# Attention and two dense networks on one core: three buffers of probabilities, and the first chunk in another order

## The chip, the cores and the metric

The kernel runs on one core of a Trainium2 chip. The metric is the device time of one execution in microseconds. Three runs of the kernel before gave 484.89, 485.83 and 486.81 us; the median, 485.83, is the number to be compared with.

## The reference

Three stages, all in float32. First a local attention with a summary of everything: 2 batches, 8 heads, 768 positions, 64 elements per head. Each query sees the keys less than 16 positions away and, beside them, 24 summary keys, one for every block of 32 (the maximum of the block's keys; the summary's value is the mean of the block's values).

```python
k_sum = k.reshape(B, H, nb, block, D).max(axis=3)
v_sum = v.reshape(B, H, nb, block, D).mean(axis=3)
scores_s = scale * np.einsum('bhsd,bhnd->bhsn', q, k_sum) + np.log(block)
scores_all = np.concatenate([np.where(mask_l, scale * (q @ k.T), -1e9), scores_s], axis=-1)
a = np.exp(scores_all - max); a = a / (sum(a) + 1e-9)
attn = a @ np.concatenate([v, v_sum], axis=2)
...
x = np.maximum(x @ w_in, 0.0) ** 2 @ w_out            # 1536 x 512 -> 2048 -> 512
...
h = x @ w_in2; solu = h * softmax(h)                  # 512 -> 1024
out = ((solu - mean) / sqrt(var + 1e-6) * g_ln) @ w_out2
```

## The kernel before, in words

**The attention.** The work is cut into 32 units (`UNITS`); a unit is a pair of heads and three tiles of 64 queries, and four units (`PPB`) with the same rows cover the four pairs of a batch. Eight units (`UPC`) give 384 tokens, a chunk; there are four chunks. A unit u goes through these steps, each a small function on the engine that does it:

- `windows_k` (GpSimd, L372) and `summaries_k` (GpSimd, L384) lay the keys of the three windows and the 24 summaries into `k_ext`; the summaries come from `sums_k` (VectorE, L593).
- `scores` (TensorE, L810): twelve small matmuls in the first chunk, three in the later ones.
- `maxima` (VectorE, L611): scale and mask into `probs[:, u % 2]` (L621), then the row maxima (L625).
- `exps` (ScalarE, L438): three exponentials in place (L443).
- `reciprocals` and `normalise` (VectorE, L628 and L635).
- `turned` (TensorE, L840): three transpositions into PSUM (L850); `copy_probsT` (ScalarE, L447) copies them to SBUF.
- `values` (TensorE, L863): twelve matmuls of the probabilities with `v_ext_first` (first chunk) or `v_ext` (L880).
- `x_high` (ScalarE, L454) and `x_low` (VectorE, L642) write the result as two parts, a high one rounded to the fast matmul format and the remainder.

The means of the first batch's values are matmuls too: `means` (L853) multiplies `v_first` by a column matrix, `copy_mean` (L465) copies the result into `v_ext_first`. Those of the second batch are made by `sums_v` and `mean_v` (L601, L606) in the steady loop and spread by DMA (`spread_v`, L267).

**The first network.** Each float32 product is three fast matmuls (high x high, high x low, low x high). For each of 16 hidden tiles f, `up` (L910, in quarters `up_part`, L897) multiplies 4 x 3 times into one PSUM bank, `hidden` makes relu and square on ScalarE (L488) and VectorE (L648), `down` (L923) multiplies 4 x 3 times by w_out. The high parts of a weight tile are made by `w_in_high` and `w_out_high` on ScalarE (L472, L476), the low parts by `w_in_low` and `w_out_low` on VectorE (L659, L664), except the first two tiles of w_in, whose low parts GpSimd makes (L392).

**The order.** Every engine has a list written out by hand for the first eight units and the first steps of the network: SyncE's requests L286 to L318, GpSimd L397 to L419, ScalarE L503 to L541, VectorE L688 to L736, TensorE L944 to L985. Waiting instructions hold up everything behind them on the same engine. TensorE's list ends with `turned(8)` and `scores(9)`; then comes the steady loop (L986), whose first product is `up(2)` and in which the later units' attention is put into slots between `up` and `down`. Some idle matmuls (`keep_busy`, L939) stand ahead of the first scores.

All loads go through one queue, in the order of the requests: keys, first queries, mask, identity, `v_first` for four pairs, `v_ext_first` in two halves (`load_vw_first`, one for each set of rows, 576 KB), and then later queries, windows of values and the weights in groups of two tiles (`load_w`).

The waits that matter here: `maxima(u)` waits for `probsT_ps` of unit u-2, since it writes into that unit's buffer; `scores(u)` waits for `masked_ok` of unit u-2 (two PSUM banks); `turned(u)` for the copy of unit u-2; `values(u)` for the mean of its pair, for `copy_probsT(u)`, for `x_low(u-2)` and, at the first unit of four, for the windows of values (`vwf_in`).

Of the kernel before, what the change touches and what calls it, by code (L numbers as in the profile page):

```python
# [7 lines left out]
F32 = mybir.dt.float32  # L8
# [71 lines left out]
def build(nc, qT, q_head, kT, vrows, vblk, vwin, vwin_head, w_in_t, w_out_t, w2_t, g_cols, mask_c, ident_c, y_dram, out):  # L80
    ctx = ExitStack()
    with ctx:
# [47 lines left out]
        v_mean = sb(att, "v_mean", [PPB * NB, P], F32)  # L130
# [3 lines left out]
        probs = sb(att, "probs", [P, 2, UC], F32)  # L134
        probsT = sb(att, "probsT", [P, 2, TPU * P], F32)
        neg_max = sb(att, "neg_max", [P, 2, TPU], F32)
        row_sum = sb(att, "row_sum", [P, 2, TPU], F32)
        row_den = sb(att, "row_den", [P, 2, TPU], F32)
        row_rec = sb(att, "row_rec", [P, 2, TPU], F32)
# [22 lines left out]
        qf_in, vwf_in = [sem(f"qf_in{i}") for i in range(3)], [sem(f"vwf_in{h}") for h in range(HPC)]  # L162
# [18 lines left out]
        win_hi_ok, win_lo_ok, win_low_ok = sem("win_hi_ok"), sem("win_lo_ok"), sem("win_low_ok")  # L181
# [67 lines left out]
        def _(sp):  # L249
# [17 lines left out]
            def spread_v(p):  # L267
                src = v_mean[p * NB:(p + 1) * NB, :].unsqueeze(1).to_broadcast([NB, TPU, P])
                sp.dma_start(v_ext[0:NB, p, :].rearrange("p (t d) -> p t d", t=TPU), src).then_inc(vs_in[p], 16)
# [13 lines left out]
            def load_vw_first(h):  # L283
                sp.dma_start(v_ext_first[NB:KX, h, :], vwin_head[h, :, :]).then_inc(vwf_in[h], 16)
# [22 lines left out]
            for u in range(UPC + 1, UPC + PPB):  # L307
                load_q(u)
                load_vw(u)
# [61 lines left out]
        def _(pool):  # L371
# [20 lines left out]
            def w_in_low(f):  # L392
                pool.wait_ge(win_hi_ok, f + 1)
                nc.gpsimd.tensor_tensor(win_lo[:, tile_cols(f)], win_raw[:, tile_cols(f)],
                                        win_hi[:, tile_cols(f)].bitcast(F32), ALU.subtract).then_inc(win_lo_ok, 1)

# [16 lines left out]
            w_in_low(1)  # L413
# [23 lines left out]
        def _(act):  # L437
            def exps(u):  # L438
                act.wait_ge(max_ok, u + 1)
                s = u % 2  # L440
# [62 lines left out]
            exps(0)  # L503
            copy_probsT(0)
            exps(1)
            exps(2)
            copy_mean(0)
            copy_mean(1)
            w_in_high(0)
            copy_probsT(1)  # L510
            w_in_high(1)
            exps(3)
            exps(4)
            copy_probsT(2)
            copy_mean(2)
            x_high(0)
            copy_probsT(3)
            x_high(1)
            exps(5)
            copy_mean(3)  # L520
            copy_probsT(4)
            x_high(2)
            exps(6)
            x_high(3)
            copy_probsT(5)
            x_high(4)
            exps(7)
            copy_probsT(6)
            x_high(5)
            w_out_high(0)  # L530
            x_high(6)
            copy_probsT(7)
            w_in_high(2)
            x_high(7)
            exps(8)
            hidden(0)
            hidden(1)
            copy_probsT(8)
            w_in_high(3)
            exps(9)  # L540
            w_out_high(1)  # L541
# [50 lines left out]
        def _(dve):  # L592
# [14 lines left out]
            def mean_v():  # L607
                dve.wait_ge(vsum_ok, VP)
                nc.vector.tensor_scalar_mul(v_mean[:, :], v_sum[:, :], 1.0 / BLOCK).then_inc(vavg_ok, 1)

            def maxima(u):  # L611
                row = u // PPB % RB
                s, kind = u % 2, 0 if row == 0 else 2 if row == RB - 1 else 1
# [5 lines left out]
                if u >= 2:  # L619
                    dve.wait_ge(probsT_ps, u - 1)  # L620
# [7 lines left out]
            def reciprocals(u):  # L628
                s = u % 2
# [5 lines left out]
            def normalise(u):  # L635
                s = u % 2
# [56 lines left out]
            reciprocals(0)  # L693
            normalise(0)
            maxima(1)
# [4 lines left out]
            reciprocals(2)  # L700
            normalise(2)
            maxima(3)
            maxima(4)
            reciprocals(3)
            normalise(3)
            reciprocals(4)
            normalise(4)
            maxima(5)
            x_low(0)
            maxima(6)  # L710
            x_low(1)
            reciprocals(5)
            normalise(5)
            x_low(2)
# [4 lines left out]
            x_low(4)  # L719
            reciprocals(7)  # L720
            normalise(7)
            x_low(5)
            x_low(6)
            maxima(8)
            x_low(7)
            w_in_low(2)
            reciprocals(8)
            normalise(8)
            hidden(0)
            w_out_low(0)  # L730
            maxima(9)
            hidden(1)
            reciprocals(9)
            normalise(9)
            w_in_low(3)
            w_out_low(1)  # L736
            for n in range(STEPS):
# [68 lines left out]
        def _(pe):  # L806
# [33 lines left out]
            def turned(u):  # L840
# [8 lines left out]
                for t in range(TPU):  # L849
                    last = nc.tensor.transpose(turned_bank(u, t), probs[:, u % 2, t * KX:(t + 1) * KX], ident[:, 0:P])  # L850
# [280 lines left out]
```

## Time and profile before

| what | before |
|---|---|
| median of three runs | 485.83 us |
| the profiled execution | 485.56 us |
| its span, first to last instruction | 483.8 us |
| TensorE busy | 474.5 us, 98% |
| VectorE busy | 254.0 us, 52% |
| ScalarE busy | 207.6 us, 43% |
| GpSimd busy | 32.8 us, 7% |

The times of rows and stretches count from the start of the span. A row of the timeline has its start, its length, engine, line, operation, output and inputs, and in brackets how long the engine was idle ahead of it and what ended that. Matmuls overlap, so the length of a group is a little more than the step from it to the next.

### The profile page before, as it was taken

The page shows a single profiled execution, that of the slowest core. Times are in us where ns is not written, and L with a number is a line of the kernel's source. Part 1 is how long each engine was busy: PE and PEld are TensorE (multiplying, and loading weights), DVE is VectorE, ACT ScalarE, POOL GpSimd, SP SyncE. Part 2 cuts the span into 40 slices and gives each one's busy share as a digit, 9 for nine tenths or more (in the row PEclk, how much of TensorE's full clock was granted, in tenths as well). Part 3 has the DMA queues.
Part 4 walks back from the last instruction along what each step waited for, and adds up shares of the span by engine and source line. Part 5 has one row for each costly group of instructions (what it writes and reads, how often), then busy time and mean ns, then how long its engine had stood idle before and what let it go on. Part 6 is the DMA issues. An engine that isn't in the chain of part 4 may idle for free.

```text
span 483.8 us, 7841 instructions
## 1 busy us (share of the span) xinstructions
PE 474.5 (98%) x2990; PEld 436.1 (90%) x2990; DVE 254.0 (52%) x515; ACT 207.6 (43%) x525; POOL 32.8 (7%) x62
## 2 busy tenths in 40 slices
PE   7899999999999999999999999999999999999997
PEld 5689999999999999999999999999888888888885
DVE  5779787985444444544443334456674444444450
ACT  3887575553534334433343323334353333333341
POOL 3420000330000000000000000000000000000000
PEclk9999999999999999999999999999999999999999
DMA  8999433222300110401000412121122000000001
GB/s 307 301 335 355 130 96 90 68 91 79 123 29 30 41 47 30 158 31 54 5 1 1 132 43 88 43 88 44 48 84 66 22 24 29 32 28 22 23 22 45
DMA packets 27270, 39.73 MB, mean 82 GB/s; under 512 B 2560, under 2 KB 16800, under 8 KB 27232
## 3 DMA queue, kind: packets, MB, share of 16 engines
q1 hardware_dynamic: 27232, 39.22, 25.0%
q8 instruction: 24, 0.39, 0.3%
q14 instruction: 14, 0.11, 0.1%
HBM read 32.77 MB, written 6.29 MB: 81 GB/s over the span
## 4 chain that ended last, share of the span: by engine, by line
PE 86%; issue 7%; DMA 2%; DVE 2%; SPq 1%; ACT 1%; POOL 0%; POOLq 0%; ACTq 0%; DVEq 0%
PE bank L933 25%; PE bank L903 25%; PE bank L1055 12%; PE bank L1028 12%; PE bank L825 4%; PE bank L880 3%; DMA v_first<-vrows 2%; PE bank L850 2%; PE bank L1043 2%; PE bank L859 1%; DVE solu L783 1%; DVE stat L775 1%; DVE lnT_lo L796 0%; SPq L251 0%; PE bank L831 0%
## 5 line engine op out<-in xcount | busy, mean ns | idle before, releaser
L903 PE MATMUL bank<-x_hi,win_hi 128*128 128x384 f32 x256 | 87.8, 343 | 0.0
L933 PE MATMUL bank<-h_hi,wout_hi 128*128 128x384 f32 x256 | 85.9, 336 | 0.0
L903 PE MATMUL bank<-x_hi,win_lo 128*128 128x384 f32 x256 | 85.8, 335 | 0.0
L933 PE MATMUL bank<-h_hi,wout_lo 128*128 128x384 f32 x256 | 85.7, 335 | 0.0
L903 PE MATMUL bank<-x_lo,win_hi 128*128 128x384 f32 x256 | 85.7, 335 | 0.0
L933 PE MATMUL bank<-h_lo,wout_hi 128*128 128x384 f32 x256 | 85.6, 334 | 0.0
L652 DVE TENSOR_TENSOR sqr<-relu 128x384 f32<-128x384 f32 x64 | 35.7, 558 | 88.1 <-ACT relu L492 87.8
L492 ACT ACTIVATE relu<-bank 128x384 f32<-128x384 f32 x64 | 31.5, 492 | 109.0 <-PE bank L903 109.0
L903 PEld LDWEIGHTS bank<-x_hi,win_hi 128*128 128x128 f32 x256 | 48.2, 188 | 0.4 <-DVE win_lo L661 0.2
L903 PEld LDWEIGHTS bank<-x_lo,win_hi 128*128 128x128 f32 x256 | 48.2, 188 | 0.0
L933 PEld LDWEIGHTS bank<-h_lo,wout_hi 128*128 128x128 f32 x256 | 48.1, 188 | 0.0
L933 PEld LDWEIGHTS bank<-h_hi,wout_hi 128*128 128x128 f32 x256 | 48.1, 188 | 0.0
L933 PEld LDWEIGHTS bank<-h_hi,wout_lo 128*128 128x128 f32 x256 | 48.1, 188 | 0.0
L903 PEld LDWEIGHTS bank<-x_hi,win_lo 128*128 128x128 f32 x256 | 48.1, 188 | 0.0
L775 DVE TENSOR_REDUCE stat<-bank 128x1 f32<-128x1024 f32 x12 | 14.7, 1225 | 49.1 <-PE bank L1028 49.1
L570 ACT ACTIVATE e_sb<-bank,stat 128x1024 f32<-128x1024 f32 x12 | 13.4, 1117 | 61.3 <-DVE stat L775 61.3
L443 ACT ACTIVATE probs<-probs,neg_max 128x120 f32<-128x120 f32 x96 | 36.5, 382 | 7.2 <-DVE neg_max L625 7.1
L1055 PE MATMUL bank<-win_hi,lnT_hi 128*128 128x512 f32 x96 | 38.4, 400 | 0.0
L656 DVE TENSOR_TENSOR h_lo<-sqr,h_hi 128x384 fp32r<-128x384 f32 x64 | 36.1, 564 | 4.2
L1055 PE MATMUL bank<-win_hi,lnT_lo 128*128 128x512 f32 x96 | 37.5, 391 | 0.0
L1055 PE MATMUL bank<-win_lo,lnT_hi 128*128 128x512 f32 x96 | 37.4, 390 | 0.0
L452 ACT COPY probsT<-bank 120x384 f32<-120x384 f32 x32 | 15.2, 476 | 45.6 <-PE bank L850 45.4
(79 smaller groups left out, 725.1 us busy)
## 6 DMA issues: line engine op xcount, KB each, us to landing
q_sb<-qT SPq DMA_DIRECT2D x24, 192.0 KB, 2.8
win_raw<-w_in_t SPq DMA_DIRECT2D x8, 512.0 KB, 11.7
wout_raw<-w_out_t SPq DMA_DIRECT2D x8, 512.0 KB, 12.4
win_raw<-w_t SPq DMA_DIRECT2D x8, 512.0 KB, 3.2
v_ext<-vwin SPq DMA_DIRECT2D x24, 144.0 KB, 2.8
k_raw<-kT SPq DMA_DIRECT2D x8, 400.0 KB, 4.0
out<-o_sb SPq DMA_DIRECT2D x12, 256.0 KB, 2.0
v_first<-vrows SPq DMA_DIRECT2D x4, 384.0 KB, 9.2
```

Source lines behind the costliest of these rows:

```text
L443: last = nc.scalar.activation(probs[:, s, c], probs[:, s, c], ACT.Exp, bias=neg_max[:, s, t:t + 1], accum_out=row_sum[:, s, t:t + 1])
L452: nc.scalar.copy(probsT[0:KX, u % 2, :], src).then_inc(probsT_ok, 1)
L492: nc.scalar.activation(relu[:, n % 2, :], up_bank(n), ACT.Relu).then_inc(relu_ok, 1)
L652: nc.vector.tensor_tensor(sqr[:, n % 3, :], relu[:, n % 2, :], relu[:, n % 2, :], ALU.mult)\
L656: nc.vector.tensor_tensor(h_lo[:, n % 3, :], sqr[:, n % 3, :], h_hi[:, n % 3, :].bitcast(F32), ALU.subtract).then_inc(hlo_ok, 1)
L775: nc.vector.tensor_reduce(stat[:, p, 0:1], h2_bank(s), AX.X, ALU.max, negate=True).then_inc(m2_ok, 1)
L825: last = nc.tensor.matmul(out_[:, t * KX:(t + 1) * KX], q_sb[:, p, t * P:(t + 1) * P], k_ext[:, p, t * KX:(t + 1) * KX], start=True, stop= ...
L880: last = nc.tensor.matmul(out_[e * D:(e + 1) * D, t * QT:(t + 1) * QT], v_tile(u, t, e), probsT[0:KX, u % 2, t * P + e * QT:t * P + (e + 1 ...
L903: last = nc.tensor.matmul(up_bank(n), win[a][:, f * WC + k * P:f * WC + (k + 1) * P], x[b][:, c % 2, k * CH:(k + 1) * CH], start=(k == 0 a ...
L933: last = nc.tensor.matmul(down_bank(d), wout[a][:, f * WC + d * P:f * WC + (d + 1) * P], h[b][:, n % 3, :], start=(f == 0 and a == 0 and b ...
L1028: last = nc.tensor.matmul(bank[:, (0, 6)[p] + half, :], y_tile(s, a, k), w2[b][:, (k * FH + half) * WC:(k * FH + half + 1) * WC], start=(k ...
L1055: last = nc.tensor.matmul(bank[:, 4 + p, :], ln[a][:, p, f * P:(f + 1) * P], w2[b][:, (F2 + f) * WC:(F2 + f + 1) * WC], start=(f == 0 and ...
```

## The change

The buffer `probs` and the four small ones beside it (`neg_max`, `row_sum`, `row_den`, `row_rec`) get three parts in place of two, and every index `u % 2` into them becomes `u % 3`; `maxima(u)` waits for the transposition of unit u-3. `v_mean` goes; `mean_v` writes `v_sum` in place and `spread_v` reads that. GpSimd's `w_in_low` goes, and VectorE makes the low parts of all tiles of w_in. `v_ext_first` is loaded in four requests (two for each set of rows, two pairs each) and `values(u)` waits for its own at each even unit. The lists of all five engines for the first chunk are put in another order, and `up_part` waits for `x_low` in front of `up(1)` too.

```diff
-        v_mean = sb(att, "v_mean", [PPB * NB, P], F32)
-        probs = sb(att, "probs", [P, 2, UC], F32)
+        probs = sb(att, "probs", [P, 3, UC], F32)
...
-        qf_in, vwf_in = [sem(f"qf_in{i}") for i in range(3)], [sem(f"vwf_in{h}") for h in range(HPC)]
+        qf_in, vwf_in = [sem(f"qf_in{i}") for i in range(3)], [sem(f"vwf_in{g}") for g in range(UPC // 2)]
...
-            def load_vw_first(h):
-                sp.dma_start(v_ext_first[NB:KX, h, :], vwin_head[h, :, :]).then_inc(vwf_in[h], 16)
+            def load_vw_first(g):
+                h, cols = g // 2, slice((g % 2) * 2 * TPU * P, (g % 2 + 1) * 2 * TPU * P)
+                sp.dma_start(v_ext_first[NB:KX, h, cols], vwin_head[h, :, cols]).then_inc(vwf_in[g], 16)
...
             load_vf(1)
+            sp.dma_start(q_first[:, 1, :], q_head[1, :, :]).then_inc(qf_in[2], 16)
             load_w(win_raw, w_in_t, 0, win_in)
-            sp.dma_start(q_first[:, 1, :], q_head[1, :, :]).then_inc(qf_in[2], 16)
             load_vw_first(0)
+            load_vw(UPC)
             load_vf(2)
-            load_vw_first(1)
             load_vf(3)
             load_q(UPC)
+            load_vw_first(1)
+            load_vw_first(2)
             sp.dma_start(mask[:, UC + KX:], mask_c[:, UC + KX:]).then_inc(edge_in, 16)
+            load_q(UPC + 1)
+            load_vw(UPC + 1)
+            load_vw_first(3)
+            load_q(UPC + 3)
+            load_w(win_raw, w_in_t, 1, win_in)
             load_w(wout_raw, w_out_t, 0, wout_in)
-            load_w(win_raw, w_in_t, 1, win_in)
-            load_vw(UPC)
-            for u in range(UPC + 1, UPC + PPB):
-                load_q(u)
-                load_vw(u)
+            load_q(UPC + 2)
+            load_vw(UPC + 3)
+            load_vw(UPC + 2)
             load_w(wout_raw, w_out_t, 1, wout_in)
...
             windows_k(0)
             summaries_k(0, 0)
+            windows_k(1)
             summaries_k(0, 1)
-            windows_k(1)
             windows_k(2)
             summaries_k(0, 2)
             windows_k(3)
+            summaries_k(0, 3)
             windows_k(4)
             windows_k(5)
-            summaries_k(0, 3)
             windows_k(6)
             windows_k(7)
-            w_in_low(0)
-            w_in_low(1)
...
-                if u >= 2:
-                    dve.wait_ge(probsT_ps, u - 1)
+                if u >= 3:
+                    dve.wait_ge(probsT_ps, u - 2)
...
-                    if p == 0:
-                        pe.wait_ge(vwf_in[row], 16)
+                    if u % 2 == 0:
+                        pe.wait_ge(vwf_in[u // 2], 16)
...
-                if f == 0:
+                if f == 0 or n == 1:
                     pe.wait_ge(xlo_ok, c * UPC + (HPC - 1) * PPB + k + 1)
```

The new lists of the three engines that compute, up to the loop (r, n, m for `reciprocals`, `normalise`, `maxima`; c for `copy_probsT`):

```
ScalarE: exps(0) exps(1) copy_mean(0) exps(2) c(0) copy_mean(1) w_in_high(0) exps(3)
 c(1) exps(4) x_high(0) exps(5) x_high(1) c(2) copy_mean(2) w_in_high(1) c(3)
 copy_mean(3) x_high(2) c(4) exps(6) x_high(3) x_high(4) c(5) exps(7) x_high(5) c(6)
 w_in_high(2) x_high(6) c(7) exps(8) x_high(7) w_out_high(0) hidden(0) w_in_high(3)
 c(8) w_out_high(1) hidden(1) exps(9)
VectorE (behind sums_k(0,2) r(0)): m(1) n(0) m(2) sums_k(0,3) r(1) n(1) r(2) m(3) n(2)
 m(4) m(5) r(3) x_low(0) n(3) r(4) n(4) r(5) n(5) m(6) w_in_low(0) x_low(1) x_low(2)
 m(7) r(6) x_low(3) n(6) x_low(4) w_in_low(1) r(7) x_low(5) n(7) m(8) x_low(6) x_low(7)
 r(8) n(8) w_in_low(2) hidden(0) w_out_low(0) m(9) w_in_low(3) r(9) n(9) w_out_low(1)
 hidden(1)
TensorE (behind scores(2)): means(0) turned(0) means(1) scores(3) turned(1) scores(4)
 scores(5) turned(2) values(0) values(1) scores(6) means(2) turned(3) means(3) values(2)
 turned(4) scores(7) values(3) values(4) turned(5) scores(8) values(5) turned(6)
 up(0) and up(1) quarter 0, values(6) turned(7), up(1) and up(0) quarter 1, values(7),
 up(1) and up(0) quarter 2, up(0) and up(1) quarter 3, turned(8) scores(9)
```

## Rows read from the trace of the kernel before

**Rows 1.** The page: busy time of TensorE, and its granted clock in 40 slices.
```profile
PE 474.5 (98%) x2990; PEld 436.1 (90%) x2990; DVE 254.0 (52%) x515; ACT 207.6 (43%) x525; POOL 32.8 (7%) x62
...
PEclk9999999999999999999999999999999999999999
```

**Rows 2.** By stretch: length, busy PE, PEld, DVE, ACT, POOL, granted clock, DMA share, GB/s.
```profile
9.87:36.16 26.29, 23.30 (x268) 19.23 (x268) 20.58 (x54) 21.24 (x76) 8.98 (x14) 1.00 1.05 326
36.16:445.00 408.84, 408.39 (x2510) 382.55 (x2509) 217.53 (x436) 173.11 (x428) 19.67 (x32) 1.00 0.21 66
```

**Rows 3.** Timeline of TensorE, four of its holes in the first chunk.
```profile
10.21 0.51 PE L850 MATMUL bank<-ident,probs 128*120 128x128 f32 x3 [0.34 <-DVE probs L639]
...
17.45 0.92 PE L880 MATMUL bank<-probsT,v_ext_first 120*64 120x64 f32 x24 [0.57 <-DMA v_ext_first<-vwin_head]
19.65 1.49 PE L859 MATMUL bank<-v_first,ident 128*24 128x128 f32 x12 [1.28 <-DMA v_first<-vrows]
...
35.22 0.52 PE L850 MATMUL bank<-ident,probs 128*120 128x128 f32 x3 [0.34 <-DVE probs L639]
```

**Rows 4.** The chain that ended last, in order of time: start, length, what.
```profile
7.56 12.04 DMA v_first<-vrows
...
21.61 0.76 PE bank L831 x12
22.37 0.47 PE bank L850 x3
22.85 1.45 PE bank L859 x12
24.30 0.50 PE bank L880 x12
...
29.00 1.06 PE bank L903 x6
```

**Rows 5.** Groups of ScalarE, 0 to 36 us: busy time, mean ns, idle time before.
```profile
L443 ACT ACTIVATE probs<-probs,neg_max 128x120 f32<-128x120 f32 x27 | 10.3, 385 | 5.9 <-DVE neg_max L625 5.8
...
L452 ACT COPY probsT<-bank 120x384 f32<-120x384 f32 x8 | 3.7, 468 | 2.1 <-PE bank L850 2.0
L469 ACT COPY v_ext_first<-bank 24x768 f32<-24x768 f32 x4 | 3.0, 782 | 2.4 <-PE bank L859 2.4
...
L474 ACT CAST win_hi<-win_raw 128x512 fp32r<-128x512 f32 x3 | 1.8, 616 | 0.0
```

**Rows 6.** Groups of VectorE, 0 to 36 us.
```profile
L639 DVE TENSOR_TENSOR probs<-probs,row_rec 128x360 f32<-128x360 f32 x9 | 5.0, 556 | 0.3
L621 DVE SCALAR_TENSOR_TENSOR probs<-bank,mask 128x360 f32<-128x360 f32 x9 | 4.8, 529 | 3.0 <-PE bank L850 1.9 <-DMA mask<-mask_c 0.7 <-PE bank L831 0.4
L625 DVE TENSOR_REDUCE neg_max<-probs 128x3 f32<-128x360 f32 x9 | 4.8, 528 | 0.3
...
L661 DVE TENSOR_TENSOR win_lo<-win_raw,win_hi 128x512 fp32r<-128x512 f32 x1 | 0.7, 681 | 0.0
```

**Rows 7.** Timeline of GpSimd: the low parts of two tiles of w_in.
```profile
15.47 2.50 POOL L394 TENSOR_TENSOR win_lo<-win_raw,win_hi 128x512 fp32r<-128x512 f32 x2 [0.35 <-ACT win_hi L474]
```

**Rows 8.** Requests (start, length) and, for each, KB and us from its start to landing.
```profile
5.20 0.71 SPq L260 DMA_DIRECT2D v_first<-vrows x1
...
v_first<-vrows SPq DMA_DIRECT2D x1, 384.0 KB, 6.4
...
8.52 0.44 SPq L260 DMA_DIRECT2D v_first<-vrows x1
...
v_first<-vrows SPq DMA_DIRECT2D x1, 384.0 KB, 14.2
...
10.42 0.47 SPq L272 DMA_DIRECT2D win_raw<-w_in_t x1
...
win_raw<-w_in_t SPq DMA_DIRECT2D x1, 512.0 KB, 16.7
```

**Rows 9.** The same by stretch: what the queue moved up to 11.6 us.
```profile
2.00:11.60 9.60, 8.04 (x61) 5.79 (x61) 6.17 (x12) 2.09 (x11) 2.93 (x9) 1.00 0.98 361
```

More of the change, by code:

```diff
@@ L503, in _ @@
             exps(0)
+            exps(1)
+            copy_mean(0)
+            exps(2)
             copy_probsT(0)
-            exps(1)
-            exps(2)
-            copy_mean(0)
             copy_mean(1)
             w_in_high(0)
+            exps(3)
             copy_probsT(1)
-            w_in_high(1)
-            exps(3)
             exps(4)
+            x_high(0)
+            exps(5)
+            x_high(1)
             copy_probsT(2)
             copy_mean(2)
-            x_high(0)
+            w_in_high(1)
             copy_probsT(3)
-            x_high(1)
-            exps(5)
             copy_mean(3)
+            x_high(2)
             copy_probsT(4)
-            x_high(2)
             exps(6)
             x_high(3)
+            x_high(4)
             copy_probsT(5)
-            x_high(4)
             exps(7)
+            x_high(5)
             copy_probsT(6)
-            x_high(5)
-            w_out_high(0)
+            w_in_high(2)
             x_high(6)
             copy_probsT(7)
-            w_in_high(2)
+            exps(8)
             x_high(7)
-            exps(8)
+            w_out_high(0)
             hidden(0)
+            w_in_high(3)
+            copy_probsT(8)
+            w_out_high(1)
             hidden(1)
-            copy_probsT(8)
-            w_in_high(3)
             exps(9)
-            w_out_high(1)
             for n in range(STEPS):
@@ L608, in mean_v @@
                 dve.wait_ge(vsum_ok, VP)
[L609 removed]
+                nc.vector.tensor_scalar_mul(v_sum[:, :], v_sum[:, :], 1.0 / BLOCK).then_inc(vavg_ok, 1)
             def maxima(u):
                 row = u // PPB % RB
[L613 removed]
+                s, kind = u % 3, 0 if row == 0 else 2 if row == RB - 1 else 1
                 if u == 0:
@@ L693, in _ @@
             reciprocals(0)
+            maxima(1)
             normalise(0)
-            maxima(1)
             maxima(2)
@@ L700, in _ @@
             reciprocals(2)
+            maxima(3)
             normalise(2)
-            maxima(3)
             maxima(4)
+            maxima(5)
             reciprocals(3)
+            x_low(0)
             normalise(3)
@@ L707, in _ @@
             normalise(4)
[L708 to L711, printed above, removed]
             reciprocals(5)
             normalise(5)
+            maxima(6)
+            w_in_low(0)
+            x_low(1)
             x_low(2)
@@ L719, in _ @@
             x_low(4)
+            w_in_low(1)
             reciprocals(7)
+            x_low(5)
             normalise(7)
-            x_low(5)
+            maxima(8)
             x_low(6)
-            maxima(8)
             x_low(7)
-            w_in_low(2)
             reciprocals(8)
             normalise(8)
+            w_in_low(2)
             hidden(0)
@@ L731, in _ @@
             maxima(9)
-            hidden(1)
+            w_in_low(3)
             reciprocals(9)
             normalise(9)
-            w_in_low(3)
             w_out_low(1)
+            hidden(1)
             for n in range(STEPS):
@@ L949, in _ @@
             scores(2)
+            means(0)
             turned(0)
-            means(0)
             means(1)
@@ L954, in _ @@
             turned(1)
-            turned(2)
             scores(4)
             scores(5)
+            turned(2)
             values(0)
             values(1)
+            scores(6)
             means(2)
             turned(3)
-            scores(6)
-            turned(4)
             means(3)
             values(2)
+            turned(4)
             scores(7)
-            turned(5)
             values(3)
             values(4)
+            turned(5)
             scores(8)
@@ L976, in _ @@
             turned(7)
+            up(1, range(1, 2))
             up(0, range(1, 2))
-            up(1, range(1, 2))
             values(7)
+            up(1, range(2, 3))
             up(0, range(2, 3))
-            up(1, range(2, 3))
             up(0, range(3, 4))
```

30 lines of the change are left out of this document (12 added, 18 removed).

## The prediction, made blind

> **What bounds the kernel now.** I read the busy shares first: TensorE is busy for 474.5 us of a span of 483.8, and its granted clock fills the whole row with nines, so it runs at 2.4 GHz throughout and only its idle time is to be had [rows 1]. The table by stretch says where that idle time lies: 2.99 us between 9.87 us (where the scores of unit 2 end) and 36.16 us (where `up(2)`, the first weight product of the steady loop, begins), and only 0.45 us in the 409 us after that [rows 2]. From 36.16 us on the loop is matmul behind matmul, so whatever is won or lost ahead of `up(2)` moves the end by as much. The idle time left lies before 9.87 us and in the second network's tail, which the edit doesn't touch. The timeline of TensorE then names the holes of the first chunk: 0.34 us for the normalised probabilities of unit 0, 0.57 us for the first windows of values (a transfer), 1.28 us for the third v_first load, and 0.34 us for the probabilities of unit 8; the rest are smaller ones of the same kinds [rows 3]. The chain of waits agrees: its largest piece ahead of `up(2)` is the transfer of v_first, 12.04 us from its request at 7.56 us to 19.60 us [rows 4].
>
> **The lengths of the steps.** On TensorE the chain's pieces give a scores step 0.76 us, a transposition (`turned`) 0.47, a mean 1.45, a values step 0.50, a quarter of an up product half of 1.06 [rows 4]. On ScalarE `exps` is three times 385 ns, 1.2 us with its read-outs; a copy of the transposed probabilities takes 0.47, a copy of a mean 0.78, a high part of a weight tile 0.62 [rows 5]. On VectorE `maxima` is 2 x 0.53, `reciprocals` with `normalise` about 0.95 (the 0.56 of the latter and two short operations, estimated at 0.2 each), a low part 0.68 [rows 6]. Neighbours on an engine overlap by up to 0.1 us.
>
> **Part 1, the requests.** All are issued by one queue, whose 16 engines are full in this stretch. The second v_first load is requested at 5.20 and lands 6.4 later, at 11.6; the fourth lands at 8.52 + 14.2 = 22.7; the second group of w_in at 10.42 + 16.7 = 27.1 [rows 8]. Up to 11.6 us the queue moves 361 GB/s [rows 9], so 384 KB cost 1.09 us and 512 KB 1.45. Between 11.6 and 22.7 us it brings 1664 KB of ordinary loads (w_in 512, q_first 384, two v_first of 384), 4.7 us at that rate; the other 6.4 us belong to 1152 KB of value windows, 1.6 us for each quarter of 288 KB, and 0.8 for the 144 KB of one later unit. With these prices the new order, from the same 11.6 us, lands so: q_first 12.7, w_in group 0 14.2, quarter 0 15.8, window of unit 8 16.6, v_first 2 and 3 17.6 and 18.7, q of unit 8 19.3, quarters 1 and 2 20.9 and 22.5, edge mask 22.7, q and window of unit 9 24.0, quarter 3 25.6, q of unit 11 26.2, w_in group 1 27.6, w_out group 0 29.1. The same sum for the kernel before would give 18.4 for the third v_first load where it landed at 19.6, and 26.3 for w_in group 1 where it was 27.1: a landing can be 1.2 us later than its sum. So each of the first chunk's transfers has this as its upper bound, and the sum as its lower.
>
> **Part 2, the walk.** Nothing changes until 9.87. Then TensorE does means(0) instead of waiting 0.34 us, to 11.3; turned(0) (normalised at 11.0, though maxima(1) now goes ahead of it), to 11.75; means(1), to 13.1. scores(3) waits for the summaries of k, which VectorE makes after maxima(2), until 13.2: **0.1 idle**. turned(1), scores(4) and (5) fill up to 15.9, where turned(2) finds norm(2) done at 15.6. ScalarE runs without a break from 10.6: exps(1), copy_mean(0), exps(2), copy_probsT(0), copy_mean(1), w_in_high(0), exps(3), and copy_probsT(1) ends at 16.9 to 17.05. values(0) is over at 16.8, so values(1) **waits 0.15**; if w_in group 0 lands at its upper bound of 15.4, w_in_high(0) starts 0.7 later and this wait is 0.6 to 0.8. I take 0.25. From there: scores(6); means(2) at 18.4, needing v_first 2 (17.6 to 18.8, so 0 to 0.4 idle; I take 0.1); turned(3) at 19.8 (norm(3) is ready at 19.3); means(3); values(2) at 21.6, with its mean at 20.8 and quarter 1 at 20.9 to 22.1 (0 to 0.5; 0.05 taken); turned(4); scores(7); values(3) at 23.3 against 22.5; values(4) at 23.8 against x_low(2) at 23.1; turned(5); scores(8); values(5) at 25.6 against copy_probsT(5) at 25.3; up parts at 26.6 against x_low(4) at 25.8 and w_in_low(1) at 26.4; values(6) at 27.6 against 27.1; turned(7) at 28.1 against 27.6; values(7) at 29.7 against 29.1; the last quarter of up(0) at 31.2 against x_low(7) at 30.9; turned(8), scores(9). All of these have 0.3 us or more in hand. Together 23.3 us of work behind 9.87 (26.29 less the 2.99 idle) and 0.5 us of these waits, plus 0.1 of the unexplained issue gaps such as the kernel has now, put `up(2)` at 33.8 instead of 36.16: **a gain of 2.4 us**. Both ends: 2.99 if no hole is left, and about 1.0 if every transfer comes at its upper bound and the waits of 0.7, 0.4 and 0.5 us, less the 0.4 already counted, don't hide each other.
>
> **Part 3, low parts on VectorE.** This takes two operations, 2.5 us together, off GpSimd [rows 7] and puts two of 0.68 on VectorE [rows 6]. Before, win_lo(0) and (1) were ready at 18 us and first wanted at 29.0 [rows 4], so nothing is won; they are now made at 22 and 25.7 us and wanted at 26.6 and 27.1. The cost is nothing while VectorE has room there; without it, up to 1.2 us. GpSimd's free time isn't wanted: its windows of k only wait for scores.
>
> **Part 4, three buffers.** maxima(u) may start when turned(u-3), not turned(u-2), is done. This alone lets exps(1), (2) and the following run before the transpositions, and so is what the walk rests on rather than a term beside it. The mean in place (`v_sum` on itself) is one operation as before, in the steady loop beside matmuls: nothing. The added wait of `up_part` in front of up(1) is for x_low of the same unit that up(0) waited for: nothing. The last operations before the loop (hidden(1) at 39.0 for a down(1) that begins at 41.5; w_out group 0 at 29.1 to 30.3 for down(0) at 35.7) have over 1 us in hand. The later weights keep their place behind the same bytes, so they land when they did and are wanted 2.4 us earlier; w_in group 1, in at 27.1 us [rows 8], had 9 us in hand at `up(2)`, and nothing waits for a later group in the 0.45 us of [rows 2].
>
> **The sum.** The profiled execution took 485.56 us, of which 483.8 are its span; 2.4 less is 483.2. It lies 0.27 below the median of the three runs, 485.83; against that I forecast 483.4.
>
> **Rivals.** *VectorE and ScalarE become the bound.* They are busy 20.58 and 21.24 us of the 26.29 [rows 2]; with 1.2 more for VectorE, in a stretch of 23.9, that is 91% and 89%. In-order queues that full rarely meet every date; for it speaks that the walk has them without a break for 10 us, against it that the margins are 0.3 to 0.8 us. Price: half of the gain, so 484.6.
> *ScalarE is blocked by w_in group 1* (the slower side). w_in_high(2) now stands ahead of x_high(6) and copy_probsT(7), which values(7) wants at 29.7. The copy of the tile, x_high(6) and the copy take 1.3 us, so the transfer has to be in by 28.4; the sum says 27.6, its upper bound 28.8 (0.4 us lost). If each request also cost the queue a fixed time, the four quarters in place of two halves would move it. From a landing of 30.8 on the whole gain is gone, and later ones make the kernel slower. Two more requests of 2 us each would put it at 31.6: 3.2 us lost against 2.4 won, 486.6. Against it: requests in a full queue land close together; v_first 3 is requested 3.3 us after v_first 1 [rows 8] and the five requests behind 11.6 land within 11.1 us, all of which their bytes explain.
> The Trainium skill (SBUF — State Buffer, "The DMA setup-cost knee") holds that every DMA pays a roughly fixed 2 us and that one should coalesce into the largest transfer. Added up in the queue this would be the last case's 486.6; the trace, where the transfers overlap, speaks against adding it up.
> *Nothing comes of it*: a dependence that I missed hands the time back before 36 us, 485.8.
>
> **How the numbers follow.** Forecast as above (a gain of 2.0 to 2.9): 0.66. Half the gain: 0.20. Nothing: 0.08. ScalarE blocked: 0.06. The range runs from 482.6 (no hole left, and a quarter of a us for the measurement) to 486.0, which takes in the second and third case. 0.5%, about what a measurement of this kernel can tell from no change, is 2.43 us, hardly more than the forecast itself: a bit over half of the first case lies beyond it, and nearly nothing of the others. So faster 0.40, same 0.55, slower 0.05.
>
> **What would show it.** In the changed profile: `up(2)` at 33.5 to 34.1 us; TensorE's idle time from 9.87 us to it under 0.9 us; no wait for v_first over 0.4 us; none for value windows; w_in_high(2) starting on its transfer at about 27.6; copy_probsT(7) over by 29.7. Wrong would be: a wait of TensorE over 0.5 us for probsT, x_lo or win_lo (the first rival), w_in group 1 landing after 28.8 (the second), or new idle time behind `up(2)`.

## The result and the profile after

Over 22 runs of each kernel on the same chips the changed one has a median of 483.34 us and the one before 486.22; the ratio is 0.9946 with a 95% interval of 0.9932 to 0.9961. That is 2.6 us (1.9 to 3.3) of 486.2, where 2.4 was forecast, and just beyond the 0.5% bound, to which I had given 0.40. One execution of the 22, at 524.9 us and a mean granted clock of 0.85, was a disturbed one and is left out of the ratio. The profiled execution took 483.07 us, with a span of 481.3.

Busy time of the changed kernel by stretch (the columns are those of [rows 2]):

```profile
0.00:9.87 9.87, 6.89 (x46) 5.25 (x48) 4.41 (x8) 2.53 (x7) 2.53 (x13) 1.00 0.81 281
9.87:36.16 26.29, 25.95 (x290) 21.98 (x287) 22.88 (x59) 23.08 (x82) 7.17 (x13) 1.00 1.06 328
36.16:445.00 408.84, 408.37 (x2505) 381.99 (x2504) 215.16 (x433) 171.54 (x423) 20.06 (x32) 1.00 0.21 67
```

The idle time of TensorE between 9.87 and 36.16 us has fallen from 2.99 us [rows 2] to 0.34, and behind it nothing has changed (0.47 against 0.45). VectorE and ScalarE, busy for 87% and 88% of these 26.29 us, have come nearer to TensorE's 99%. Ahead of 9.87 us this execution has 2.98 us idle. The timeline of TensorE says where (start, length, what, and in brackets the idle time ahead and what ended it):

```profile
8.83 1.45 PE L831 MATMUL bank<-k_ext,q_first 64*64 64x120 f32 x24 [0.94 <-DMA q_first<-q_head]
10.21 1.49 PE L859 MATMUL bank<-v_first,ident 128*24 128x128 f32 x12
...
17.56 0.57 PE L880 MATMUL bank<-probsT,v_ext_first 120*64 120x64 f32 x12 [0.29 <-ACT probsT L450]
18.06 0.83 PE L831 MATMUL bank<-k_ext,q_first 64*64 64x120 f32 x12
18.82 1.49 PE L859 MATMUL bank<-v_first,ident 128*24 128x128 f32 x12
...
32.67 0.49 PE L850 MATMUL bank<-ident,probs 128*120 128x128 f32 x3
32.99 0.83 PE L825 MATMUL bank<-k_ext,q_sb 128*128 128x120 f32 x6
```

None of the four holes of [rows 3] is there. Behind 10.21 us one named wait is left: values(1), for copy_probsT(1). scores(9) at 32.99 is the last work ahead of `up(2)`, which begins 0.60 later, at 33.59 (in the kernel before, 36.16). The query load for scores(1) came 0.4 us later in this execution than in the one before, by chance: the requests ahead of it are the same. So the fairer measure is the stretch from the end of scores(2) (here the start of means(0), 10.21) to `up(2)`: **23.4 us in place of 26.3**. I call it the first chunk's stretch below.

Two dates of ScalarE, from its timeline:

```profile
15.29 0.62 ACT L472 CAST win_hi<-win_raw 128x512 fp32r<-128x512 f32 x1 [0.34 <-DMA win_raw<-w_in_t]
...
27.39 0.62 ACT L472 CAST win_hi<-win_raw 128x512 fp32r<-128x512 f32 x1
28.56 0.32 ACT L461 CAST x_hi<-bank 128x192 fp32r<-128x192 f32 x1 [0.54 <-PE bank L880]
29.02 0.48 ACT L450 COPY probsT<-bank 120x384 f32<-120x384 f32 x1
```

w_in group 0 landed at about 15.2, 1.0 us behind the sum and just inside its upper bound (15.4), and the copy of its first tile waited 0.34 us for it. Group 1 was in before ScalarE asked for it at 27.39, and copy_probsT(7) was over at 29.5.

### The profile page after: what moved, and what is told of

It reads as the page before. It is cut to its first block, busy times and chain, and to the rows that moved or that the text cites. A ratio compares the mean times of both kernels' runs of the same rounds, so it can differ in the third digit from the quotient of the medians.

```text
span 481.3 us, 7844 instructions
## 1 busy us (share of the span) xinstructions
PE 474.0 (98%) x2990; PEld 436.1 (91%) x2990; DVE 253.7 (53%) x517; ACT 207.4 (43%) x525; POOL 30.9 (6%) x60
## 4 chain that ended last, share of the span: by engine, by line
PE 86%; issue 7%; DVE 2%; DMA 2%; SPq 1%; ACT 1%; POOL 0%; POOLq 0%; ACTq 0%; DVEq 0%
PE bank L903 25%; PE bank L931 25%; PE bank L1053 13%; PE bank L1026 12%; PE bank L825 4%; PE bank L880 3%; PE bank L1041 2%; PE bank L850 2%; DMA win_raw<-w_in_t 2%; PE bank L859 1%; DVE solu L783 1%; DVE stat L775 1%; DVE lnT_lo L796 0%; SPq L250 0%; PE bank L831 0%
## 5 line engine op out<-in xcount | busy, mean ns | idle before, releaser
L650 DVE TENSOR_TENSOR sqr<-relu 128x384 f32<-128x384 f32 x64 | 35.7, 558 | 88.2 <-ACT relu L490 87.9
L494 ACT ACTIVATE h_hi<-relu 128x384 fp32r<-128x384 f32 x64 | 33.7, 527 | 2.0
## 6 DMA issues: line engine op xcount, KB each, us to landing
wout_raw<-w_out_t SPq DMA_DIRECT2D x8, 512.0 KB, 12.7
```

The lines of the kernel that those rows point to most:

```text
L494: nc.scalar.activation(h_hi[:, n % 3, :], relu[:, n % 2, :], ACT.Square).then_inc(hhi_ok, 1)
L650: nc.vector.tensor_tensor(sqr[:, n % 3, :], relu[:, n % 2, :], relu[:, n % 2, :], ALU.mult)\
```

## The experiments

All ratios are against the kernel before, on the same chip, with 95% intervals. "Stretch" is the first chunk's, from the one profiled execution of each run; the reason for it is below (the start varies by up to 2.3 us between executions). Where scores(2) is done late, the transfers and the other engines have had more time, so waits for them are shorter: a stretch behind 11.2 us or later flatters the kernel a little.

| run | ratio | scores(2) done | `up(2)` | stretch |
|---|---|---|---|---|
| before | 1 | 9.87 | 36.16 | 26.3 |
| changed | 0.9946 (0.9932 to 0.9961) | 10.21 | 33.59 | 23.4 |
| e1 requests alone | 0.9966 (0.9947 to 0.9985) | 11.44 | 36.4 | 25.0 |
| e2 three buffers alone | 1.0004 (0.9978 to 1.0029) | 10.1 | 35.7 | 25.6 |
| e3 both | 0.9973 (0.9952 to 0.9994) | 12.1 | 38.6 | 26.4 |
| e4 changed, old requests | 0.9961 (0.9943 to 0.9980) | 9.93 | 34.9 | 25.0 |
| e5 changed, two buffers | 1.0155 (1.0127 to 1.0182) | 11.33 | 45.4 | 34.1 |
| e6 changed, low parts on GpSimd | 0.9958 (0.9935 to 0.9981) | 9.93 | 34.7 | 24.8 |
| e7 changed, eight requests | 0.9937 (0.9916 to 0.9959) | 11.23 | 34.6 | 23.4 |
| e8 changed, w_in group 1 late | 1.0011 (0.9985 to 1.0036) | 11.86 | 36.4 | 24.5 |
| e9 as e6, but later on GpSimd | 0.9970 (0.9954 to 0.9986) | 11.43 | 34.7 | 23.3 |
| e10 pairs, two idle matmuls | 0.9960 (0.9942 to 0.9977) | 10.10 | 33.2 | 23.1 |
| e11 pairs, one idle matmul | 0.9949 (0.9929 to 0.9969) | 9.96 | 33.1 | 23.1 |
| e12 five idle matmuls first | 0.9970 (0.9947 to 0.9994) | 11.62 | 36.2 | 24.5 |

**e1, the requests alone.** The kernel before with the changed kernel's list of requests and its four quarters.

```diff
             load_vf(1)
+            sp.dma_start(q_first[:, 1, :], q_head[1, :, :]).then_inc(qf_in[2], 16)
             load_w(win_raw, w_in_t, 0, win_in)
-            sp.dma_start(q_first[:, 1, :], q_head[1, :, :]).then_inc(qf_in[2], 16)
             load_vw_first(0)
+            load_vw(UPC)
             load_vf(2)
-            load_vw_first(1)
...
```

> The kernel before with the new requests alone (order, quarters). Theory: two of the holes, 0.57 us for the first value windows and 1.28 us for the third v_first load, are filled by the transfers alone, since these now land at about 15.9 and 17.8 us; up(2) begins at 34.3 to 34.7 us instead of 36.16, the time falls by 1.5 to 1.9 us (0.3 to 0.4%). The holes for the probabilities of units 0, 2 and 8 (0.3 us each) stay. Rival: the old lists, with two buffers, are bound by VectorE and ScalarE as soon as the transfers come; then most of it comes back as waits for probsT or norm and up(2) stays behind 35.5.

1.65 us (0.7 to 2.6) were gained, as forecast. `up(2)`, at 36.4, is not where it was forecast (34.3 to 34.7), mostly because this execution's scores(2) ended 1.6 us late; its stretch would put `up(2)` at 34.9. And the two transfer holes were not all: a new one came. Timelines of ScalarE and TensorE:

```profile
30.85 0.62 ACT L486 CAST wout_hi<-wout_raw 128x512 fp32r<-128x512 f32 x1 [1.78 <-DMA wout_raw<-w_out_t]
31.38 0.31 ACT L469 CAST x_hi<-bank 128x192 fp32r<-128x192 f32 x1
```
```profile
32.22 0.57 PE L886 MATMUL bank<-probsT,v_ext_first 120*64 120x64 f32 x12 [0.79 <-DVE x_lo L651]
```

w_out group 0, now requested behind more, lands at 30.8, and the old list has `w_out_high(0)` ahead of x_high(6): 1.78 us of ScalarE, 0.79 of TensorE. The request order and ScalarE's list belong together: the new requests with the old list leave this wait, and e4 below has the opposite case.

**e2, three buffers alone.**

```diff
-        probs = sb(att, "probs", [P, 2, UC], F32)
+        probs = sb(att, "probs", [P, 3, UC], F32)
...
-                if u >= 2:
-                    dve.wait_ge(probsT_ps, u - 1)
+                if u >= 3:
+                    dve.wait_ge(probsT_ps, u - 2)
...
```

> The kernel before with three buffers of probabilities alone (mean in place too). Theory: maxima(5) no longer waits 1.9 us for the transposition of unit 3, but TensorE waited for transfers there, so up(2) stays at 36.0 to 36.2 and the time within 0.2 us. Rival: the third buffer is what brings the gain; then up(2) is before 35 us.

No effect (1.0004). `up(2)` at 35.7 lies outside what I had written, since v_first 2 landed 0.5 us sooner in this execution (the wait for it was 0.76 us in place of 1.28); the other holes stood.

**e3, both.** The old lists on the computing engines, new requests, three buffers.

> The kernel before with the new requests and three buffers, old lists on the computing engines. Theory: as with the requests alone, up(2) at 34.3 to 34.7, since the old lists are written for two buffers; the last 0.7 to 1.0 us to the changed kernel's 33.6 are the lists'. Rival: the buffers and the requests are enough, up(2) by 33.9.

1.3 us gained (0.3 to 2.3), no more than with the requests alone: the buffers add nothing to the old lists. Its profiled execution had a late query load: TensorE stood still for 2.28 us, and the granted clock was then 0.50 from 11 to 14 us, which is why `up(2)` is at 38.6. It was not the only one: four of its twelve executions have a mean clock of 0.995 or 0.996 and took 486.9 to 488.3 us, the other eight at most 485.4.

**e4, the changed kernel with the old requests.**

```diff
+            load_w(win_raw, w_in_t, 0, win_in)
             sp.dma_start(q_first[:, 1, :], q_head[1, :, :]).then_inc(qf_in[2], 16)
-            load_w(win_raw, w_in_t, 0, win_in)
             load_vw_first(0)
-            load_vw(UPC)
+            load_vw_first(1)
             load_vf(2)
+            load_vw_first(2)
+            load_vw_first(3)
             load_vf(3)
...
```

> The changed kernel with the old order of requests (the quarters of the value windows side by side in place of each half). Theory: v_first 2 lands at 19.6 and v_first 3 at 22.7 again, so TensorE, which has its other work done sooner, waits about 0.4 us for the value windows, 0.5 to 1.2 us ahead of means(2) and about 1 us ahead of means(3); up(2) at 35.3 to 35.9, the time 0.4 to 0.8 us under the kernel before. Rival: the lists carry the gain, up(2) by 34.5.

The hole moved to the fourth v_first load, as the timeline of TensorE shows:

```profile
17.20 0.57 PE L877 MATMUL bank<-probsT,v_ext_first 120*64 120x64 f32 x12 [0.19 <-ACT probsT L447]
...
22.01 1.49 PE L856 MATMUL bank<-v_first,ident 128*24 128x128 f32 x12 [1.59 <-DMA v_first<-vrows]
```

1.6 us in one piece, where I had 1.9 to 2.6 in three; `up(2)` at 34.9 and 1.9 us gained (1.0 to 2.8) are better than the 0.4 to 0.8 forecast. The forecast had v_first 2 land at 19.6, as in the kernel before; it landed at 18.2, with the halves of the value windows split into quarters in front of it. Whether the split or chance did that isn't shown. All but the requests (lists, buffers and low parts) and the requests alone are each worth over half of the whole, and the sum of both (3.5) is more than the 2.6 of the two together, though not beyond the intervals.

**e5, two buffers.** `maxima(5)` must then go behind `normalise(4)`, or the engines wait for each other in a ring.

```diff
-        probs = sb(att, "probs", [P, 3, UC], F32)
+        probs = sb(att, "probs", [P, 2, UC], F32)
...
-                if u >= 3:
-                    dve.wait_ge(probsT_ps, u - 2)
+                if u >= 2:
+                    dve.wait_ge(probsT_ps, u - 1)
...
             maxima(4)
-            maxima(5)
             reciprocals(3)
             x_low(0)
             normalise(3)
             reciprocals(4)
             normalise(4)
+            maxima(5)
```

> The changed kernel with two buffers; maxima(5) has to go behind normalise(4) on VectorE, everything else stays. Theory: maxima(5) now waits for the transposition of unit 3 (about 20.7 us instead of 17.0), exps(5) on ScalarE with it, and x_high(1), copy_probsT(2), copy_mean(2) stand behind exps(5) in the same queue; values(2), at 22.1 in the changed kernel, waits for the mean until 24.3, so up(2) comes 2.0 to 2.5 us later, at 35.6 to 36.1, and the whole gain but 0.3 us is gone. Rival: the buffers don't matter with the new transfers, up(2) stays by 34.0.

The hole ahead of values(2) is as forecast (2.42 us), and yet the kernel is 7.5 us slower than before and 10 slower than the changed one. First the timeline of TensorE, then its stretches:

```profile
15.72 0.83 PE L831 MATMUL bank<-k_ext,q_first 64*64 64x120 f32 x12 [1.00 <-POOL k_ext L394]
...
23.51 1.49 PE L859 MATMUL bank<-v_first,ident 128*24 128x128 f32 x12
27.42 0.91 PE L880 MATMUL bank<-probsT,v_ext_first 120*64 120x64 f32 x12 [2.42 <-ACT v_ext_first L467]
28.26 0.90 PE L850 MATMUL bank<-ident,probs 128*120 128x128 f32 x3
29.08 1.47 PE L831 MATMUL bank<-k_ext,q_first 64*64 64x120 f32 x12
```
```profile
24.00:26.00 2.00, 1.00 (x10) 0.69 (x7) 0.75 (x2) 1.18 (x7) 0.00 (x0) 1.00 1.05 276
26.00:28.00 2.00, 0.58 (x11) 0.61 (x12) 0.87 (x3) 2.00 (x6) 0.00 (x0) 0.76 1.05 356
28.00:30.00 2.00, 2.00 (x20) 1.54 (x18) 0.70 (x2) 1.59 (x4) 1.04 (x1) 0.50 1.09 280
...
40.00:42.00 2.00, 2.00 (x17) 1.74 (x17) 0.36 (x1) 1.45 (x6) 0.00 (x0) 0.83 1.08 357
42.00:44.00 2.00, 2.00 (x22) 1.93 (x21) 1.14 (x5) 1.28 (x6) 0.00 (x0) 1.00 1.05 314
```

After the 2.42 us without work the granted clock (third number from the right) goes from 1.00 to 0.50, that is from 2.4 to 1.2 GHz, and is back only at 42 us: a values step takes 0.91 us in place of 0.57, twelve scores 1.47 in place of 0.83. Two things were missed. One is a second wait: maxima(2) has to wait for turned(0) too (0.92 us of VectorE), the summaries of unit 3 stand behind it, and scores(3) waits 1.00 us for them. The other is the clock. TensorE is idle for 5.5 us of the stretch in place of 0.34 (all its waits and gaps together), and busy for 28.6 us in place of 23.0 with the same work: of the 10.7 us lost, about half is idle time and half are matmuls at the lower clock. All six executions of this run have a mean clock of 0.993 or less. So the third buffer is needed by these lists, by far more than the one wait that was forecast; that no other list could do with two isn't shown.

**e6, low parts on GpSimd again.**

```diff
             windows_k(7)
+            w_in_low(0)
+            w_in_low(1)
             windows_k(UPC)
...
             maxima(6)
-            w_in_low(0)
             x_low(1)
...
             x_low(4)
-            w_in_low(1)
             reciprocals(7)
...
```

> The changed kernel with the low parts of w_in tiles 0 and 1 on GpSimd again (behind windows of unit 7). Theory: VectorE had room, so up(2) stays within 0.2 us of 33.6 and the time within 0.3 us of the changed kernel's. Rival (VectorE as the bound): taking 1.2 us of work off it brings up(2) forward by 0.3 us or more; or slower copies and a shared read path cost it as much.

The stretch grew by 1.4 us, to 24.8. The theory is out; of the rival, its second half had it, the shared read path, though not with this size. Timelines of GpSimd, VectorE and TensorE:

```profile
15.39 1.26 POOL L399 TENSOR_TENSOR win_lo<-win_raw,win_hi 128x512 fp32r<-128x512 f32 x1 [0.35 <-ACT win_hi L479]
```
```profile
15.43 1.61 DVE L644 TENSOR_TENSOR probs<-probs,row_rec 128x360 f32<-128x360 f32 x1
...
26.32 1.11 DVE L644 TENSOR_TENSOR probs<-probs,row_rec 128x360 f32<-128x360 f32 x1
```
```profile
17.18 0.52 PE L855 MATMUL bank<-ident,probs 128*120 128x128 f32 x3 [1.20 <-ACT probsT L457]
...
27.59 0.52 PE L855 MATMUL bank<-ident,probs 128*120 128x128 f32 x3 [0.51 <-DVE probs L644]
```

normalise(2) begins 0.04 us after GpSimd's subtraction and takes 1.61 us, not 0.52: it is held up by most of the time until GpSimd ends, at 16.65. turned(2) then comes 1.20 us late (the profile names copy_probsT as the releaser; norm(2), at 17.04, is what came last before 17.18). A second meeting, with GpSimd's copies delayed by the other low part, costs normalise(6) 0.6 and TensorE 0.51. The Trainium skill (SBUF — State Buffer, "Who interferes with whom") says that a VectorE instruction with two SBUF inputs contends with a GpSimd instruction that reads SBUF, and that whoever issues first holds the shared ports for the whole instruction. The trace agrees: 1.09 us lost beside a 1.26 us operation that began first. In the runs' times the 1.4 us can't be seen: 0.9958 lies within the changed kernel's interval and the other way round.

**e9, the same later on GpSimd.** The two subtractions behind windows_k(9).

> The changed kernel with the low parts of tiles 0 and 1 on GpSimd, but behind its windows of units 8 and 9 rather than ahead of them. In the run with them ahead, normalise(2) took 1.61 us in place of 0.52 while GpSimd made the first low part, and 24.8 us went by from the end of scores(2) (9.93) to up(2) (34.73), against 23.4 in the changed kernel. Theory (a VectorE operation with two inputs in SBUF is held up while GpSimd reads there): here GpSimd's 1.26 us fall beside maxima(4) and (5), which read PSUM and one SBUF tensor or one tensor alone; no normalise in the first chunk takes over 0.8 us, and the stretch is 23.3 to 23.7 us. Rival (VectorE's load, or where GpSimd's work delays its windows): the stretch stays at 24.3 us or more.

```profile
18.05 1.27 POOL L399 TENSOR_TENSOR win_lo<-win_raw,win_hi 128x512 fp32r<-128x512 f32 x1
22.88 1.27 POOL L399 TENSOR_TENSOR win_lo<-win_raw,win_hi 128x512 fp32r<-128x512 f32 x1 [3.56 <-ACT win_hi L479]
```

Both fall beside maxima and x_low, which have one input in PSUM or only one at all; no normalise takes over 0.74 us, and the stretch is 23.3. So in these profiles it is the meeting that costs, not the engine that does the work; VectorE's relief isn't worth anything either. That rests on the rows of one execution each: by the runs' times e9 (0.9970) and e6 (0.9958) don't differ, and e9 is if anything slower than the changed kernel, by 1.2 us, give or take 1.1, which its profile doesn't explain. So that GpSimd can do this work later at no cost is not shown. The profiled execution of e9 has the late start described below, which flatters its stretch.

**e7, eight requests.**

```diff
-                h, cols = g // 2, slice((g % 2) * 2 * TPU * P, (g % 2 + 1) * 2 * TPU * P)
-                sp.dma_start(v_ext_first[NB:KX, h, cols], vwin_head[h, :, cols]).then_inc(vwf_in[g], 16)
+                h = g // 2
+                for i in range(2):
+                    at = (g % 2) * 2 + i
+                    cols = slice(at * TPU * P, (at + 1) * TPU * P)
+                    sp.dma_start(v_ext_first[NB:KX, h, cols], vwin_head[h, :, cols]).then_inc(vwf_in[2 * g + i], 16)
...
-                    if u % 2 == 0:
-                        pe.wait_ge(vwf_in[u // 2], 16)
+                    pe.wait_ge(vwf_in[u], 16)
```

> The changed kernel with the value windows of the first chunk in eight requests, one for each unit, in the places of the four; the same bytes. Theory: requests in a full queue overlap and only bytes cost, w_in group 1 lands at 27.1 plus or minus 0.4 and the time stays within 0.3 us. Rival (a fixed cost for each request, 2 us): four more requests put v_first 2 two us and w_in group 1 eight us later, and the kernel is slower than the one before by over 2 us.

The load of w_in group 1, with its KB and us from request to landing:

```profile
win_raw<-w_in_t SPq DMA_DIRECT2D x1, 512.0 KB, 12.7
```

Requested at 14.90, it lands 12.7 later, at 27.6, half a us later than in the changed kernel with four requests more; the stretch is the same 23.4. A cost of 2 us added up for each request is out.

**e8, w_in group 1 late.**

```diff
-            load_w(win_raw, w_in_t, 1, win_in)
             load_w(wout_raw, w_out_t, 0, wout_in)
             load_q(UPC + 2)
             load_vw(UPC + 3)
             load_vw(UPC + 2)
+            load_w(win_raw, w_in_t, 1, win_in)
```

> The changed kernel with w_in group 1 requested behind w_out group 0 and the queries and windows of units 10 and 11, so that it lands at 30.9 to 31.3 us instead of 27.1. Theory (the price of the slower rival): w_in_high(2) blocks ScalarE until then, values(7) waits for copy_probsT(7) until about 32.3 instead of beginning at 29.98, and up(2) comes 2.2 to 2.6 us later, at 35.8 to 36.2. Rival: ScalarE catches up, since its work ahead of values(7) is short; under 1 us lost.

```profile
31.31 0.62 ACT L472 CAST win_hi<-win_raw 128x512 fp32r<-128x512 f32 x1 [2.24 <-DMA win_raw<-w_in_t]
```
```profile
32.67 0.57 PE L880 MATMUL bank<-probsT,v_ext_first 120*64 120x64 f32 x12 [1.07 <-DVE x_lo L643]
```

The whole gain is gone (1.0011): 3.2 us against the changed kernel, give or take 1.4, where 2.2 to 2.6 was forecast. The executions are of two kinds, which was not forecast: the six with a mean clock of 0.999 or more have a median of 485.6 us, five with 0.992 to 0.996 took 487.8 to 489.6 (the sixth of these 486.4), where the changed kernel has one such clock in 21. A longer wait of TensorE with the loss of clock seen in e5 would explain them, but none of them was profiled. The mechanism of the slower rival is real; the change only keeps clear of it. The stretch, 24.5, shows 1.1 of it alone, since scores(2) ended 1.6 us late in this execution and TensorE had that much less time to wait.

**e10 to e12, the start.** The runs above fall into executions in which scores(2) ends at 9.9 to 10.2 and others at 11.2 to 12.1. In the second kind (here e7) the scores of unit 0 and three idle matmuls run at half the rate of the first (here the changed kernel: 0.83 and 1.56 us):

```profile
5.60 1.47 PE L834 MATMUL bank<-k_ext,q_first 64*64 64x120 f32 x12 [0.72 <-POOL k_ext L397]
7.00 2.93 PE L942 MATMUL bank<-idle 128*128 128x256 f32 x6
```

In e3 and e12 it was the query load for scores(1) that came late, by about 1.5 us. Where TensorE is the bound from 10 us on, each costs its full length. e10 and e11 try to do without both:

```diff
-            sp.dma_start(q_first[:, 0, 0:UQ], q_head[0, :, 0:UQ]).then_inc(qf_in[0], 16)
+            sp.dma_start(q_first[:, 0, 0:2 * UQ], q_head[0, :, 0:2 * UQ]).then_inc(qf_in[0], 16)
...
-                if u in (0, 1, PPB):
-                    pe.wait_ge(qf_in[min(u, 2)], 16)
+                if u in (0, 2, PPB):
+                    pe.wait_ge(qf_in[u // 2], 16)
...
-            keep_busy(3)
             scores(1)
+            keep_busy(2)
...
+            maxima(1)
             reciprocals(0)
-            maxima(1)
             normalise(0)
```

> The changed kernel with the first query request holding pairs 0 and 1 (192 KB) and the second pairs 2 and 3, scores(1) right behind scores(0) with two idle matmuls behind it in place of three ahead, and maxima(1) ahead of reciprocals(0). Theory: TensorE is the bound from scores(2) on, so what counts is when scores(2) ends: about 10.2 us where the idle matmuls run at the full clock (10.2 in the changed kernel), about 10.9 where they run at half of it (11.2 there), and executions with a late query load, which end 3 us later, go away. Median 0 to 0.6 us under the changed kernel's. Rival: ScalarE and VectorE, which get their work sooner, are the bound; then the stretch behind scores(2) shrinks too.

> As the one before, with one idle matmul. Theory: scores(2) ends by 10.3 us at either clock, 0.3 to 0.8 us under the changed kernel in the median. Rival: the longer idle time before scores(2), 1.5 us or more, lets the granted clock fall, as after the 2.3 us without work in the run with both requests and buffers; then it is slower than with two.

> The changed kernel with five idle matmuls at the very start in place of four. Theory: matmuls run at half rate until the clock rises, which in some executions comes only at 9.8 us; more work ahead of scores(0) makes it come by 6 us in most, at 0.1 to 0.4 us for scores(0), which nothing waits for. The median falls by 0.3 to 0.8 us. Rival: when the clock rises doesn't hang on it, and the time is the same or 0.3 us longer.

e11 ended scores(2) at 9.96 and `up(2)` began at 33.1, the earliest of all; 1.38 us without work did not lower its clock. But the ratios 0.9960 and 0.9949 are the changed kernel's 0.9946 within their intervals, and the profiled executions were both of the kind that starts early, so the gain of up to 0.5 us is seen in a profile and not shown in the times. The rival of e10 came true beside the theory: the stretch shrank by 0.3 us in both, to 23.1. The wait of values(1) for copy_probsT(1), 0.29 us, is gone; in e10 w_in_high(0) begins at 14.71, in the changed kernel at 15.29, where ScalarE waited 0.34 us for the load of w_in group 0. The executions that end 2 to 3 us late did not go away: one of ten in each run has a mean clock of 0.996, at 485.3 and 485.8 us. e12 had the clock up by 6.6 us, but a late query load; its 0.9970 shows no gain.

## Why the prediction was right

**The sum.** Forecast 2.4 us, measured 2.6 (1.9 to 3.3). `up(2)` was to begin at 33.5 to 34.1 and began at 33.59; TensorE's idle time behind 9.87 was to be under 0.9 and is 0.34; w_in_high(2) was to start at 27.6 and did at 27.4; copy_probsT(7) was over at 29.5. Per stretch the gain was 2.9, half a us more than I had. Half of that are waits: those for the summaries (0.1), for v_first 2 (0.1) and for quarter 1 (0.05) did not come, and values(1) waited 0.29 where 0.25 was taken. The other half I had not forecast: TensorE's busy time in the stretch is 23.04 us, not 23.3. The 0.34 us of the late query load took some of it back in the profiled execution, so part of the closeness of 33.59 to the forecast 33.8 is luck. w_in_high(2) did not start on its transfer, as I had written: the tile was in 0.3 us before. The lower end of the gain was added up wrongly: 2.4 less 0.7, 0.4 and 0.5 plus 0.4 is 1.2, not 1.0. And "at 2.4 GHz throughout" holds for the record of the clock only: the first eight idle matmuls of the kernel before took 3.78 us, 0.47 each, and six later ones 1.56, 0.26 each.

**Part 1, the requests.** The prices, 361 GB/s for ordinary loads and 1.6 us for a quarter of the value windows, gave w_in group 1 at 27.6; it landed at 27.1 (12.77 + 14.3), and group 0 at 15.2, within its bound. Six requests landed between 11.6 and 22.7, not five, and since the 1.6 us was got from these same landings, that their bytes explain them was no test; the new order was one, and v_first 2 and 3 landed at 17.4 and 18.2 where the sum had 17.6 and 18.7. e1 shows that this part alone brings most of the gain, and e4 that the rest without it brings about as much. That the parts overlap, since each fills time that the other would, was not said.

**Part 3 was wrong.** "Nothing is won" by moving the low parts to VectorE: e6 shows 1.4 us of the stretch, in its profile. I costed the two subtractions by their dates and by VectorE's room, and not by what stands beside them. In the kernel before, the same GpSimd operations [rows 7] ran beside the maxima of units 3 and 4 and the first operation of reciprocals(3), which took 0.53 us where others take 0.15, and this loss was hidden by the transfer holes; in the new order they would have met normalise(2), on which TensorE waits. The sum came out right because the walk used normalise's undisturbed length throughout, which only holds with this part in; that was luck. e9's rows say that the cost is the meeting's.

**Part 4, three buffers.** The walk rests on them, as said: alone they do nothing (e2), but the new lists without them lose everything (e5). That the loss would be four times the forecast wait, half of it through the clock, I had not weighed anywhere: the walk's holes were priced at their length.

**The rivals.** VectorE and ScalarE are at 87% and 88% and hardly bound: taking two operations of 0.68 us off VectorE (e9) left the stretch at 23.3 (its time was no better), and ScalarE's share is the 0.29 us that are gone in e10. The slower side, ScalarE blocked by w_in group 1, works as priced (e8), and its trigger, a fixed cost for each request, isn't there (e7). "Nothing comes of it" is out.

**The chances.** Faster beyond 0.5% had 0.40 and came, by 0.04% more than the bound; the interval holds both sides of the bound, so on which side the change lies is not shown.

## What to carry to other kernels

When the work ahead of a steady loop is reordered, the order of requests and each engine's list are one thing: moved alone, either left a wait of 0.8 to 1.6 us here (e1, e4). Before an operation stays on GpSimd, look at what VectorE does at that time: here a two-input operation from SBUF took 1.61 us in place of 0.52 beside GpSimd's subtraction (e6). And price an idle stretch of TensorE not by its length alone: behind the 2.42 us of e5 the clock went too, and cost as much again as all the idle time.

## What the runs showed of the hardware

- The granted clock fell to 0.50 after 2.42 us (e5) and 2.28 us (e3) without work and stayed there for some 14 and 3 us; after 2.05 us (e12) and 1.38 us (e11) it stayed at 1.00.
- At the start of an execution matmuls run at half rate while the record of the granted clock reads 1.00 (e7, 7.00 us: 2.93 us for what takes 1.56). When this ends varies between executions whose work on TensorE is the same up to there, from before 5.6 us (the changed kernel) to about 9.8 us (e7). Why was not found.
- The value windows, which go into 96 partitions, cost about twice as much as loads into 128 for the same bytes. This is an estimate from the landings of [rows 8] and the rate of [rows 9]: 1.6 us for 288 KB against 1.09 for 384. With it the landings came within 1.2 us of their sums, whether each half came in one, two or four requests (before, changed, e7). That the number of partitions is the reason isn't shown; no run changed it alone.
